# Moving eight of twelve attention chunks in between the matmul groups of the first expert layer

## The chip, the cores and the metric

The kernel runs on one core of one Trainium2 chip. The metric is the device time of one execution in microseconds (us); lower is better. All engines of the core run side by side, each through its own list of instructions: TensorE (PE, its weight loads are PEld), VectorE (DVE), ScalarE (ACT), GpSimd (POOL) and SyncE (SP), which here only issues DMAs. They are tied together by semaphores that the kernel sets and waits on by hand.

## What is computed

Three stages in a row, all in 32-bit floats. A gated recurrent attention (2 sequences, 8 heads, 768 steps, head size 40) gives rows `x` (1536 x 320), and two expert layers follow it, each a pair of 320 x 1536 projections multiplied with each other and a 1536 x 320 projection back:

```python
for t in range(S):
    m_new = np.maximum(f_gate[:, :, t] + m, i_gate[:, :, t])
    f_stab, i_stab = np.exp(f_gate[:, :, t] + m - m_new), np.exp(i_gate[:, :, t] - m_new)
    C = f_stab * C + i_stab * outer(vt, kt)        # one 40 x 40 state for each head
    n = f_stab * n + i_stab * kt
    y[:, :, t] = sigmoid(o_gate[:, :, t]) * (C @ qt) / max(|n . qt|, 1)
x = y as rows (1536 x 320)
x = (sigmoid(x @ w_gate) * (x @ w_val)) @ w_out    # first expert layer
x = ((x @ w_a) * (x @ w_b)) @ w_out2               # second expert layer
```

## The kernel before

**Attention.** The sequences are cut into chunks of 128 steps, 12 in all (`NCH`), numbered n = 2i + p with p the sequence. The gate sums and running maxima of all chunks are made at the start by DVE, on rows of 16 partitions (`gate_sums`, `gate_max`). For each chunk PE then makes these pieces:

- `spread` (L328): the weights' exponents of 8 heads, as 3 + 3 matmuls into a PSUM bank, one of each pair for the triangular mask (L340) and one that copies two rows of `arow` to all partitions (L350). The first chunk takes the rows from SBUF instead, with 8 small matmuls (L346).
- `scores` (L360): 3 matmuls, 1024 columns of f32.
- `from_state` (L370) and `values` (L381): the part out of the carried state `cst` and the part of the chunk itself, 8 small matmuls. They go into two banks, and DVE joins them.
- `to_state` (L393): what the chunk adds to the state.
- `turn` (L403): 3 transposes of the finished rows.

ACT makes `exp` of what `spread` wrote (`weigh`, L566), DVE multiplies with the scores (`product`, L768), joins the parts and divides (`combine`, L785 to L800), and updates the state (`state`, L775 and L778). POOL scales `v` (`weigh_v`, L894), decays the state (`decay`, L913) and multiplies with the opened output gate (`open_x`, L902 and L904). ACT and DVE then split the turned rows into a high and a low part in `xt` (`x_high` L189, `x_low` L194 and L196). The order on each engine is written out: in `step(i, p)` PE runs the first pieces of the next chunk around the last pieces of this one.

**Expert layers.** Each layer has 3 groups of 512 rows (`NG`) and 12 slices of the hidden size (`NF`): 72 units in both layers. In a unit, `up` makes two sums of 8 matmuls of 512 columns (L465), into `GB` and `VB`, which have two banks each; ACT (`gate`, L638 and L641) and DVE (`hidden`, L839 and L841) make of them `h_hi` and `h_lo`; `down` makes 12 matmuls of 320 columns (L482) into four banks `OB`. PE runs `up` of the next unit ahead of `down`. Between the layers the rows are copied to `x_next` and turned with 12 transposes a group (L513). The weights come as 24 tiles of 544 KB by DMA and are split into `w_hi` by ACT (L579, L586) and `w_lo` by POOL (L919). All tiles of the first layer are split in a fixed order from chunk 0 on; the first layer starts when the rows of the first four chunks are in `xt` (L531) and all but the end of the last chunk is done (L530 to L545).

Of the kernel before, what the change touches and what calls it, by code (L numbers as in the profile page):

```python
# [33 lines left out]
TRI = 3 * HD  # L34
KREM = DM - 2 * P
# [7 lines left out]
RING = 4  # L43
LATE = 5
EARLY = 6
THIRDS = ((0, 3), (3, 3), (6, 2))
LOW = -1.0e30
BIG = 2.0 ** 100


def wait(eng, sem, value):

    if not (isinstance(value, int) and value <= 0):
        eng.wait_ge(sem, value)


def build(nc, f_in, i_in, q_in, kq3_in, vk_in, o_in, w1_in, w2_in, consts_in, bm_in, out):
    ctx = ExitStack()
    with ctx:
# [5 lines left out]


# [8 lines left out]
        w_hi_late = sb("w_hi_late", [P, LATE * WC], F32R)  # L75
        w_hi = sb("w_hi", [P, (NF - LATE) * WC], F32R)
        w_lo = sb("w_lo", [P, EARLY * WC], F32R)
        opened = ExitStack()
        osig = opened.enter_context(nc.sbuf_tensor("osig", [P, NCH * DM], F32))
        opened.close()  # L80
        w_lo_late = sb("w_lo_late", [P, (NF - EARLY) * WC], F32R)
        xt = sb("xt", [P, 5 * TOK], F32R)
        w_raw0 = sb("w_raw0", [P, WC])
        consts = sb("consts", [P, 2 * P])
        ident = consts[:, 0:P]


        att = ExitStack()

        def ab(name, shape, dt=F32):  # L90
            return att.enter_context(nc.sbuf_tensor(name, shape, dt))

        q_blk = [ab(f"q_blk{i}", [TRI, HEADS * P]) for i in range(2)]
        k3 = [ab(f"k3_{i}", [TRI, 3 * P]) for i in range(2)]
        q3 = [ab(f"q3_{i}", [TRI, 3 * P]) for i in range(2)]
        arow = [ab(f"arow{i}", [P, HEADS * P], F32R) for i in range(2)]
        vk = [ab(f"vk_{i}", [P, VALL + 3 * TRI]) for i in range(2)]
        d_row = ab("d_row", [ROWS, CHUNKS])
        m_prev = ab("m_prev", [ROWS, CHUNKS])
        wt = ab("wt", [P, HEADS * P])  # L100
        pt = [ab(f"pt{i}", [P, HEADS * P]) for i in range(2)]
        u_num = ab("u_num", [P, VALL])
        x_raw = [ab(f"x_raw{i}", [P, DM]) for i in range(2)]
        x_n = [ab(f"x_n{i}", [P, 3 * P]) for i in range(2)]
        v_w = ab("v_w", [P, VALL])
        cst = [ab(f"cst{i}", [TRI, VALL]) for i in range(2)]
        t_st = ab("t_st", [TRI, VALL])
        bmask = ab("bmask", [TRI, VALL])
        g_col = ab("g_col", [P, NCH * HEADS])
        i_col = ab("i_col", [P, NCH * HEADS])  # L110
        w_col = ab("w_col", [P, NCH * HEADS])
        dec = ab("dec", [TRI, NCH * HEADS])
        den = [ab(f"den{i}", [P, HEADS]) for i in range(2)]
        rec = [ab(f"rec{i}", [P, HEADS]) for i in range(2)]
        ones = ab("ones", [P, P], F32R)
        consts_r = ab("consts_r", [P, 2 * P], F32R)
        ident_r, ahead = consts_r[:, 0:P], consts_r[:, P:2 * P]
        att.close()


        w_raw = [w_raw0, sb("w_raw1", [P, WC])]
        h_hi = [sb(f"h_hi{i}", [P, TG], F32R) for i in range(RING)]
        h_lo = [sb(f"h_lo{i}", [P, TG], F32R) for i in range(RING)]
        s_ff = [sb(f"s_ff{i}", [P, TG]) for i in range(2)]
        h_ff = [sb(f"h_ff{i}", [P, TG]) for i in range(2)]
        x_next = [sb(f"x_next{i}", [P, 3 * P]) for i in range(BLK)]
        y_out = [sb(f"y_out{i}", [P, DM]) for i in range(BLK)]

        bank = [ctx.enter_context(nc.psum_tensor(f"bank{i}", [P, 512], F32)) for i in range(8)]
        AB, OA, OI, SC, TP, ST = bank[0], bank[1], bank[4], bank[5], bank[6], (bank[2], bank[3], bank[7])  # L130
        GB, VB, OB = [bank[0], bank[2]], [bank[1], bank[3]], bank[4:8]

        a_dram = nc.dram_tensor("a_scratch", [2, CHUNKS * ROWS * P], F32, kind="Internal").ap()
        d_dram = nc.dram_tensor("d_scratch", [ROWS, CHUNKS], F32, kind="Internal").ap()

        (ld_gate, ld_ident, ld_bmask, st_rows, st_dec, ld_dec) = (
            sem(n) for n in ("ld_gate", "ld_ident", "ld_bmask", "st_rows", "st_dec", "ld_dec"))
        ld_o = [sem(f"ld_o{i}") for i in range(4)]
        ld_q, ld_a, ld_v = ([sem(f"ld_{x}{i}") for i in range(2)] for x in "qav")
        ld_w = [sem(f"ld_w{i}") for i in range(2)]  # L140
        (dve_gate, dve_split, dve_rows, dve_const, pe_cols, act_cols, act_osig, act_dec) = (
            sem(n) for n in ("dve_gate", "dve_split", "dve_rows", "dve_const", "pe_cols", "act_cols",
                             "act_osig", "act_dec"))
        (ab_ready, st_ready, act_exp, dve_p, pool_v, pe_av, pe_inter, pe_state) = (
            sem(n) for n in ("ab_ready", "st_ready", "act_exp", "dve_p", "pool_v", "pe_av",
                             "pe_inter", "pe_state"))
        (dve_t, pool_cd, dve_c, dve_u, dve_num, dve_den, dve_rec, dve_y, pool_x, pe_turn, act_xhi,
         dve_xlo) = (sem(n) for n in (
             "dve_t", "pool_cd", "dve_c", "dve_u", "dve_num", "dve_den", "dve_rec", "dve_y", "pool_x",
             "pe_turn", "act_xhi", "dve_xlo"))  # L150
        act_whi, pool_wlo, pool_zero, pool_lo = (
            sem(n) for n in ("act_whi", "pool_wlo", "pool_zero", "pool_lo"))
        (pe_g, pe_v, act_s, dve_h, act_hhi, dve_hlo, pe_mm2, pe_ob, act_next, dve_next, pe_tr, act_tr, dve_tr,
         act_y, dve_yo, st_out) = (sem(n) for n in (
             "pe_g", "pe_v", "act_s", "dve_h", "act_hhi", "dve_hlo", "pe_mm2", "pe_ob", "act_next", "dve_next",
             "pe_tr", "act_tr", "dve_tr", "act_y", "dve_yo", "st_out"))
# [11 lines left out]
        def w_part(low, f, at=0, k=WC):  # L168

            if low:  # L170
                tile, f = (w_lo, f) if f < EARLY else (w_lo_late, f - EARLY)
            else:
                tile, f = (w_hi, f) if f < NF - LATE else (w_hi_late, f - (NF - LATE))
            return tile[:, bass.ds(f * WC + at, k)]

        def w_buf(m, f):

            return 0 if m == 0 and f < EARLY else f % 2

        def w_landed(m, f):  # L180

            before = (EARLY if f % 2 == 0 else 0) + (NF - EARLY) // 2 * m
            return ld_w[f % 2], 16 * (before + (f - (EARLY if m == 0 else 0)) // 2 + 1)

        xt3 = xt[:, :].rearrange("p (j t) -> p j t", t=TOK)

        def split_high(act, bank_, at):

            return act.copy(xt3[:, 0::2, bass.ds(at, P)], bank_[:, 0:3 * P].rearrange("p (j t) -> p j t", t=P))  # L189
# [820 lines left out]
```

## Time and profile before

| | |
|---|---|
| median of 3 runs | 488.54 us (488.37 to 488.55) |
| the profiled execution | 488.71 us |
| its span, first to last instruction | 486.6 us |
| PE busy | 475.3 us (98%) |
| DVE, ACT, POOL busy | 190.9, 162.9, 95.6 us |
| moved by DMA | 28.90 MB, 59 GB/s over the span |

The page gives busy time as a share of the span. A PE that is busy all the time is not yet a PE at its peak, since matmuls are pipelined and their ends are modelled; so what a matmul costs is read from one start to the next. The profile's clock row (PEclk) is the share of the 2.4 GHz that was granted.

### The profile page before, as it was taken

The numbers are of one execution on the slowest core, as the hardware profiler recorded it, in microseconds if no ns is written. First come the engines' busy times: TensorE is split into PE (matmuls) and PEld (weight loads), VectorE is DVE, ScalarE is ACT, GpSimd is POOL, SyncE is SP. The second block draws the span as 40 slices with busy tenths as digits, with TensorE's granted clock in tenths as the row PEclk, the third lists the DMA queues.
The fourth block names the chain that finished last, engine by engine and source line by source line (L and its number), as shares of the span: only waits on it lengthen the run. The fifth ranks groups of instructions, "written<-read, shape, count | busy, mean of one in ns | idle before, by whom it ended". The sixth has DMA issues, their size and how long they took to land.

```text
span 486.6 us, 7131 instructions
## 1 busy us (share of the span) xinstructions
PE 475.3 (98%) x2587; PEld 417.3 (86%) x2587; DVE 190.9 (39%) x369; ACT 162.9 (33%) x320; POOL 95.6 (20%) x77
## 2 busy tenths in 40 slices
PE   4999999999999999999999999999999999999997
PEld 3788888888888888888988888888888888888886
DVE  8479999732222622224422235222232222222223
ACT  4555555434422422223333445222232222222222
POOL 1356666424500000000055443200000000000000
PEclk9999999999999999999999999999999999999999
DMA  7656655142310000000022331000010000100001
GB/s 253 173 167 180 191 189 165 46 139 90 95 47 0 2 0 1 0 1 0 1 92 93 100 129 49 1 0 1 0 55 0 1 0 1 54 1 1 1 0 54
DMA packets 15729, 28.90 MB, mean 59 GB/s; under 512 B 1850, under 2 KB 10530, under 8 KB 15702
## 3 DMA queue, kind: packets, MB, share of 16 engines
q1 hardware_dynamic: 15702, 28.53, 19.0%
q8 instruction: 18, 0.29, 0.3%
q14 instruction: 9, 0.07, 0.1%
HBM read 26.47 MB, written 2.05 MB: 59 GB/s over the span
## 4 chain that ended last, share of the span: by engine, by line
PE 93%; DVE 2%; DMA 1%; POOL 1%; issue 1%; SPq 1%; POOLq 0%; DVEq 0%
PE bank L465 54%; PE bank L482 26%; PE bank L381 3%; PE bank L360 3%; PE bank L370 1%; PE bank L393 1%; PE bank L340 1%; PE bank L403 1%; DMA q_blk<-q_in 1%; PE bank L350 1%; PE bank L513 1%; DVE m_row L722 1%; POOL w_lo L919 1%; POOL a_lo L926 0%; DMA d_scratch<-d_row 0%
## 5 line engine op out<-in xcount | busy, mean ns | idle before, releaser
L465 PE MATMUL bank<-xt,w_hi 128*128 128x512 f32 x420 | 137.5, 392 | 0.0
L839 DVE TENSOR_TENSOR h_ff<-bank,s_ff 128x512 f32<-128x512 f32 x72 | 49.8, 692 | 223.4 <-PE bank L465 211.3
L465 PE MATMUL bank<-xt,w_hi_late 128*128 128x512 f32 x300 | 97.9, 391 | 0.0
L641 ACT CAST h_hi<-h_ff 128x512 fp32r<-128x512 f32 x72 | 44.6, 620 | 143.6 <-DVE h_ff L839 143.6
L465 PEld LDWEIGHTS bank<-xt,w_hi 128*128 128x128 f32 x420 | 77.0, 188 | 13.9
L638 ACT ACTIVATE s_ff<-bank 128x512 f32<-128x512 f32 x72 | 43.1, 598 | 128.1 <-PE bank L465 128.0
L465 PE MATMUL bank<-xt,w_lo 128*128 128x512 f32 x216 | 84.1, 389 | 0.0
L465 PE MATMUL bank<-xt,w_lo_late 128*128 128x512 f32 x216 | 84.0, 389 | 0.0
L841 DVE TENSOR_TENSOR h_lo<-h_ff,h_hi 128x512 fp32r<-128x512 f32 x72 | 49.8, 692 | 49.3 <-ACT h_hi L641 49.3
L465 PEld LDWEIGHTS bank<-xt,w_hi_late 128*128 128x128 f32 x300 | 55.1, 188 | 9.9
L919 POOL TENSOR_TENSOR w_lo<-w_raw,w_hi 128x1088 fp32r<-128x1088 f32 (+1 forms) x12 | 31.5, 2622 | 122.7 <-ACT w_hi L586 122.7
L482 PE MATMUL bank<-w_hi,h_lo 128*128 128x320 f32 x168 | 51.9, 309 | 0.0
L482 PE MATMUL bank<-w_hi,h_hi 128*128 128x320 f32 x168 | 51.7, 308 | 0.0
L465 PEld LDWEIGHTS bank<-xt,w_lo 128*128 128x128 f32 x216 | 40.6, 188 | 8.8
L465 PEld LDWEIGHTS bank<-xt,w_lo_late 128*128 128x128 f32 x216 | 40.6, 188 | 8.7
L482 PE MATMUL bank<-w_lo,h_hi 128*128 128x320 f32 x144 | 44.4, 309 | 0.0
L482 PE MATMUL bank<-w_lo_late,h_hi 128*128 128x320 f32 x144 | 44.4, 309 | 0.0
L566 ACT ACTIVATE wt<-bank,g_col 128x128 f32<-128x128 f32 x96 | 28.6, 367 | 33.7 <-PE bank L350 32.5
L482 PE MATMUL bank<-w_hi_late,h_lo 128*128 128x320 f32 x120 | 37.1, 309 | 0.0
L482 PE MATMUL bank<-w_hi_late,h_hi 128*128 128x320 f32 x120 | 36.9, 308 | 0.0
L482 PEld LDWEIGHTS bank<-w_hi,h_hi 128*128 128x128 f32 x168 | 31.5, 188 | 1.4
L919 POOL TENSOR_TENSOR w_lo_late<-w_raw,w_hi_late 128x1088 fp32r<-128x1088 f32 x10 | 25.3, 2532 | 32.7 <-ACT w_hi_late L586 32.7
(88 smaller groups left out, 513.2 us busy)
## 6 DMA issues: line engine op xcount, KB each, us to landing
w_raw<-w_in SPq DMA_DIRECT2D x24, 544.0 KB, 3.6
vk<-vk_in SPq DMA_DIRECT2D x12, 344.0 KB, 3.4
k<-kq_in SPq DMA_DIRECT2D x12, 180.0 KB
q<-kq_in SPq DMA_DIRECT2D x12, 180.0 KB, 2.8
osig<-o_in SPq DMA_DIRECT2D x4, 480.0 KB, 5.4
y<-y_out SPq DMA_DIRECT2D x12, 160.0 KB, 1.8
q_blk<-q_in SPq DMA_DIRECT2D x24, 60.0 KB
q_blk<-q_in SPq DMA_DIRECT2D x12, 40.0 KB
```

Source lines behind the costliest of these rows:

```text
L340: pe.matmul(ab[:, 0:k * P], ident_r, ahead.unsqueeze(1).to_broadcast([P, k, P]), start=True, stop=False)
L350: pe.matmul(ab[:, 0:k * P], ones[:, :], arow[p][:, h * P:(h + k) * P], start=False, stop=True).then_inc(ab_ready, 1)
L360: pe.matmul(ST[x][:, 0:k * P], k3[p][:, x * P:(x + 1) * P], q_blk[p][:, h * P:(h + k) * P], start=True, stop=True).then_inc(st_ready, 1)
L381: mm = pe.matmul(OA[:, h * VW:(h + 1) * VW], pt[p][:, h * P:(h + 1) * P], vk[p][:, h * VW:(h + 1) * VW], start=True, stop=True)
L465: mm = pe.matmul(banks[f % 2][:, :], w_part(low, f, (gv * 3 + kt) * P, P), xt[:, bass.ds(xb * TOK + g * TG, TG)], start=(j == 0), stop=(j ...
L482: mm = pe.matmul(OB[tb][:, 0:DM], h[r][:, tb * P:(tb + 1) * P], w_part(low, f, W1C, DM), start=(f == 0 and j == 0), stop=(f == NF - 1 and ...
L566: a = act.activation(wt[:, h * P:(h + 1) * P], ab[:, j * P:(j + 1) * P], ACT.Exp, scale=-1.0, bias=g_col[:, bass.ds(n * HEADS + h, 1)])
L638: act.activation(s_ff[f % 2][:, :], GB[f % 2][:, :], fn).then_inc(act_s, 1)
L641: act.copy(h_hi[f % RING][:, :], h_ff[f % 2][:, :]).then_inc(act_hhi, 1)
L839: dve.tensor_tensor(h_ff[f % 2][:, :], VB[f % 2][:, :], s_ff[f % 2][:, :], ALU.mult).then_inc(dve_h, 1)
L841: dve.tensor_tensor(h_lo[f % RING][:, :], h_ff[f % 2][:, :], h_hi[f % RING][:, :].bitcast(F32), ALU.subtract).then_inc(dve_hlo, 1)
L919: pool.tensor_tensor(w_part(1, f), w_raw[0 if early else w_buf(m, f)][:, :], w_part(0, f).bitcast(F32), ALU.subtract).then_inc(pool_wlo, 1)
```

## The change

Four chunks (`ALONE`) run before the first expert layer starts, and the other eight are cut into three pieces each, which PE issues between the two halves of `up` and behind `down` in units 0 to 22 of the first layer's 36. One chunk takes three units. What else is different:

- `spread` is 2 matmuls of 512 columns: the mask stands in the rows of `arow` itself (filled once from `consts`), and a matrix `sel` picks them. The first chunk goes the same way, with its rows fetched by DMA.
- `q` is multiplied on POOL with a row of gate factors (`scale_q`, rows made by ACT in `i_rows`, stored to DRAM and fetched back three times over), so `from_state` and `values` add up in one bank, and `combine` on DVE has one product less and no sum.
- The gate factors' columns (`i_col`, one `columns` set of three) are gone.
- PSUM: `GB` and `VB` have one bank each, `OB` four, and two banks `XY` serve the pieces of attention. The SBUF tiles of one chunk exist once for the eight interleaved chunks and twice for the four alone.
- The output gate is opened for 4 chunks at once at the start, and for the others one by one.
- Every loop is unrolled; `w_raw` has three buffers; the weights are split at units given by `W_AT`.
- The next group's rows for the second layer are turned piecewise (`turn_rows`, at the units of `next_turns` and behind chunks 8 to 11), and `h_hi`, `h_lo` have two buffers in place of four.

The core of the diff: PE's pieces and order, then the order of ACT, of DVE and of POOL.

```diff
+UNITS = 2 * NG * NF
+ALONE = 4
+RING = 3
...
+def set_of(n):
+    return n % 2 if n < ALONE else 0
...
+def piece(u):
+    n, k = divmod(u + 1, 3)
+    n += ALONE
+    return (n, k) if n < NCH else (None, None)
...
+        GB, VB, OB, XY = bank[0], bank[1], bank[2:6], bank[6:8]
...
+            def spread(n):
+                s = set_of(n)
+                pe.wait_ge(ld_a[s], 32 + 16 * use_of(n))
+                for half in range(2):
+                    if n <= ALONE:
+                        wait(pe, act_e, 2 * n - 1 + half)
+                    elif half == 0:
+                        pe.wait_ge(dve_xlo, n)
+                    else:
+                        wait(pe, dve_c, n if last_with_state(n - 1) else 0)
+                        wait(pe, dve_tr, n - 8)
+                    pe.matmul(XY[half][:, :], sel[:, :], arow[s][:, half * HALF:(half + 1) * HALF],
+                              start=True, stop=True).then_inc(pe_ab, 1)
...
+            def values(n):
+                s, p = set_of(n), n % 2
+                acc = value_bank(n)
+                if n >= BATCH:
+                    pe.wait_ge(dve_y, n - 1)
+                    pe.wait_ge(dve_c, n - 1)
+                    pe.wait_ge(pool_q, n - 1)
+                    if n >= ALONE:
+                        pe.wait_ge(dve_p, 2 * n + 1)
+                    for x, (h, k) in enumerate(((0, 3), (3, 3), (6, 2))):
+                        mm = pe.matmul(acc[:, h * VW:(h + k) * VW], q3[s][:, x * P:(x + 1) * P],
+                                       cst[p][:, h * VW:(h + k) * VW], start=(x == 0), stop=False)
+                    mm.then_inc(pe_f, 1)
...
+            spread(1)
+            scores(1, 0)
+            scores(1, 1)
+            values(0)
+            columns(range(1, CHUNKS), 0, dve_gate, 9)
+            columns(range(1, CHUNKS), 1, dve_rows, 3)
+            to_state(0)
+            spread(2)
+            scores(2, 0)
+            scores(2, 1)
+            pe.wait_ge(act_cols, 4)
+            turn(0)
+            values(1)
+            to_state(1)
+            spread(3)
+            scores(3, 0)
+            scores(3, 1)
+            turn(1)
+            values(2)
+            spread(4)
+            values(3)
+            to_state(2)
+            to_state(3)
+            scores(4, 0)
+            turn(2)
+            scores(4, 1)
+            turn(3)
...
+            for u in range(UNITS - 1):
+                n, k = piece(u)
+                up(u, 0)
+                if k == 0:
+                    spread(n)
+                if k == 1 and n > ALONE:
+                    scores(n, 0)
+                    scores(n, 1)
+                if k == 2 and last_with_state(n):
+                    to_state(n)
+                up(u, 1)
+                if k == 2:
+                    turn(n)
+                    if n >= NCH - BLK:
+                        turn_rows(0, n - (NCH - BLK))
+                for g, tb in next_turns(u):
+                    turn_rows(g, tb)
+                if u == UNITS - 2:
+                    up(u + 1, 0)
+                    up(u + 1, 1)
+                if u:
+                    down(u - 1)
+                if k == 1:
+                    values(n)
...
+            weigh(0, 0)
+            weigh(0, 1)
+            i_rows()
+            weigh(1, 0)
+            weigh(1, 1)
+            w_high(0)
+            gate_cols(1)
+            act.wait_ge(ld_dec, 16)
+            act.activation(dec[:, :], dec[:, :], ACT.Exp).then_inc(act_dec, 1)
+            act.wait_ge(act_cols, 3)
+            weigh(2, 0)
+            weigh(2, 1)
+            x_high(0)
+            w_high(1)
+            weigh(3, 0)
+            weigh(3, 1)
+            x_high(1)
+            w_high(2)
+            weigh(4, 0)
+            weigh(4, 1)
+            x_high(2)
+            x_high(3)
+            w_high(3)
...
+            W_AT = {0: (4,), 1: (5, 6), 3: (7,), 4: (8, 9), 6: (10,), 7: (11,)}
+            for u in range(UNITS):
+                n, k = piece(u)
+                gate(u)
+                if k == 0:
+                    weigh(n, 0)
+                if k == 1:
+                    open_gate(n)
+                h_high(u)
+                if k == 0:
+                    weigh(n, 1)
...
+            state(0)
+            product(2, 0)
+            product(2, 1)
+            x_low(0)
+            combine(1)
+            state(1)
+            product(3, 0)
+            product(3, 1)
+            x_low(1)
+            combine(2)
+            combine(3)
+            state(2)
+            state(3)
+            product(4, 0)
+            x_low(2)
+            x_low(3)
+            product(4, 1)
...
+            for u in range(UNITS):
+                n, k = piece(u)
+                if k == 1 and n > ALONE:
+                    product(n, 0)
+                    product(n, 1)
+                if k == 2:
+                    combine(n)
+                    if last_with_state(n):
+                        state(n)
+                hidden(u)
+                h_low(u)
...
+            pool.wait_ge(act_cols, 2)
+            weigh_v(0)
+            weigh_v(1)
+            w_low(0)
+            open_x(0)
+            pool.wait_ge(act_cols, 4)
+            scale_q(2)
+            weigh_v(2)
+            w_low(1)
+            open_x(1)
+            decay(2)
+            scale_q(3)
+            weigh_v(3)
+            open_x(2)
+            decay(3)
+            open_x(3)
+            w_low(2)
+            scale_q(4)
+            weigh_v(4)
+            w_low(3)
```

SP issues its DMAs one after the other too. Ahead of the interleaved part its order is: gate rows, constants, output gate, `q`, `v` of chunk 0, `q` of chunk 1, the four `arow` rows of chunks 0 and 1 (which wait for the masks and for DVE), `v` of chunk 1, the mask, weight tile 0; then the stores of the exponent rows (after POOL's `a_lo`), the store of the gate factors (after ACT's `i_rows`), `q` and the rows of chunk 2, the store and the fetch of the decays (`dec`) with the scaled `q` of chunk 2 between them, and `v` 2, rows and `q` 3, tile 1, and so on.

## Rows read from the trace of the kernel before

**Rows 1.** The page's first part: busy us, share of the span and instructions.
```profile
PE 475.3 (98%) x2587; PEld 417.3 (86%) x2587; DVE 190.9 (39%) x369; ACT 162.9 (33%) x320; POOL 95.6 (20%) x77
```

**Rows 2.** Timeline of PE in the attention stage: start us, us, what.
```profile
31.62 1.89 PE L360 MATMUL bank<-q_blk,k 120*128 120x384 f32 x6
33.16 0.53 PE L340 MATMUL bank<-consts_r 128*128 128x384 f32 x1
```

**Rows 3.** Timeline of PE at the start of the first expert layer.
```profile
86.79 0.70 PE L465 MATMUL bank<-xt,w_hi 128*128 128x512 f32 x2
...
87.56 0.62 PE L465 MATMUL bank<-xt,w_hi 128*128 128x512 f32 x2
...
88.71 0.79 PE L370 MATMUL bank<-cst,q 120*128 120x123 f32 x6
89.34 1.92 PE L381 MATMUL bank<-vk,pt 128*128 128x41 f32 x16
91.08 0.53 PE L403 MATMUL bank<-consts,x_n 128*128 128x128 f32 x3
```

**Rows 4.** Chain of work that ended last: start us, us, what; attention, then expert units.
```profile
31.78 1.72 PE bank L360 x6
...
104.59 3.65 PE bank L465 x16
108.24 1.75 PE bank L482 x12
...
162.31 1.31 PE bank L513 x12
```

**Rows 5.** Timelines of DVE and of POOL at the start.
```profile
4.83 0.41 DVE L713 TENSOR_TENSOR_SCAN s_row<-rst,f_row 16x128 f32<-16x128 f32 x1
...
12.95 0.48 DVE L753 CAST a_hi<-m_row 16x640 fp32r<-16x640 f32 x1
...
13.51 2.12 POOL L926 TENSOR_TENSOR a_lo<-m_row,a_hi 16x640 fp32r<-16x640 f32 x1 [10.93 <-DVE a_hi L753]
```

**Rows 6.** DMA from 15 to 40 us: what, size, median us to landing.
```profile
w_raw<-w_in SPq DMA_DIRECT2D x2, 544.0 KB, 4.3
...
dec<-d_scratch SPq DMA_DIRECT2D x1, 45.0 KB, 3.8
```

**Rows 7.** Timeline of ACT.
```profile
13.05 2.17 ACT L566 ACTIVATE wt<-bank,g_col 128x128 f32<-128x128 f32 x8
...
30.17 1.10 ACT L579 CAST w_hi<-w_raw 128x1088 fp32r<-128x1088 f32 x1
...
92.20 1.28 ACT L638 ACT_TABLE_LOAD   x1
```

**Rows 8.** Timelines of DVE and of POOL in one chunk.
```profile
64.64 0.17 DVE L792 SCALAR_TENSOR_TENSOR den<-u_num 128x8 f32<-128x8 f32 x1
...
65.79 0.55 DVE L768 TENSOR_TENSOR pt<-bank,wt 128x384 f32<-128x384 f32 x1
66.26 0.41 DVE L194 TENSOR_TENSOR xt<-bank,xt 128x256 f32 x1
...
67.01 0.92 DVE L768 TENSOR_TENSOR pt<-bank,wt 128x384 f32<-128x384 f32 x2
...
66.06 0.32 POOL L902 TENSOR_TENSOR x_n<-x_raw,osig 128x64 f32<-128x64 f32 x1 [2.85 <-DVE x_raw L800]
66.35 0.87 POOL L904 TENSOR_TENSOR x_n<-x_raw,osig 128x320 f32<-128x320 f32 x1
```

**Rows 9.** Timelines of POOL and of DVE at 70 us.
```profile
69.08 2.75 POOL L919 TENSOR_TENSOR w_lo<-w_raw,w_hi 128x1088 f32 x1
...
70.46 1.41 DVE L792 SCALAR_TENSOR_TENSOR den<-u_num 128x8 f32<-128x8 f32 x1
```

**Rows 10.** Timeline of PE at 13 us, and busy time by stretch at the end.
```profile
13.27 3.78 PE L360 MATMUL bank<-q_blk,k 120*128 120x384 f32 x6
...
484.50:486.60 2.10, 0.00 (x0) 0.00 (x0) 0.00 (x0) 0.00 (x0) 0.00 (x0) 0.71 0.50 173
```

More of the change, by code:

```diff
@@ L294, in _ @@
[L294 to L307 removed]
+            sp.dma_start(dec[:, :], d_dram.rearrange("r c -> (r c)").partition_broadcast(TRI)).then_inc(ld_dec, 16)
@@ new lines, in scores @@
+            def scores(n, half):
+                s = set_of(n)
+                pe.wait_ge(ld_q[s], 64 * (use_of(n) + 1))
+                if n < ALONE:
+                    wait(pe, dve_p, 2 * n - 1 + half)
+                elif n == ALONE:
+                    pe.wait_ge(dve_y, n - 1 + half)
+                else:
+                    pe.wait_ge(act_e, 2 * n + half + 1)
+                st = score_bank(n, half)
+                for h, k in (((0, 3), (3, 1)), ((4, 2), (6, 2)))[half]:
+                    at = (h - half * HEADS // 2) * P
+                    x = h // 3
+                    mm = pe.matmul(st[:, at:at + k * P], k3[s][:, x * P:(x + 1) * P],
+                                   q_blk[s][:, h * P:(h + k) * P], start=True, stop=True)
+                mm.then_inc(pe_s, 1)
@@ L548, in _ @@
-            run(0, NG - 1, after_turn(NG - 1), 0, "next")
-            run(1, 0, after_turn(NG), 1, True)
-            with pe.Fori(1, NG - 1) as g:
-                run(1, g, after_rows(g), g + 1, False)
-            run(1, NG - 1, after_rows(NG - 1), None, False)
+                mm.then_inc(pe_d, 1)
+            pe.wait_ge(ld_ident, 16)
+            columns(range(1), 0, dve_gate, 5)
+            columns(range(1), 1, dve_rows, 1)
+            scores(0, 0)
+            scores(0, 1)
+            pe.wait_ge(pool_sel, 4)
@@ L872, in _ @@
[L872 to L884 removed]
+            product(1, 0)
+            product(1, 1)
+            combine(0)
+            dve.wait_ge(ld_bmask, 16)
@@ new lines, in _ @@
+            for u in range(3 * (NCH - ALONE) - 1):
+                n, k = piece(u)
+                if k == 0 and n > ALONE:
+                    scale_q(n)
+                    if last_with_state(n):
+                        weigh_v(n)
+                if k == 2:
+                    if last_with_state(n):
+                        decay(n)
+                    open_x(n)
+                for f in W_AT.get(u, ()):
+                    w_low(f)
+            for f in range(NF):
+                w_low(NF + f)
```

1065 lines of the change are left out of this document (443 added, 622 removed).

## The prediction, made before the changed kernel was run

> **What bounds the kernel now.** I read the page's first part first. PE is busy 475.3 of 486.6 us, the other engines at most 191 [rows 1]. So only what PE executes, or a wait of PE, can move the end. The timeline of PE then shows two regimes. Up to 86.8 us it runs the twelve chunks, each piece starting where the one before ends [rows 2]; from there on it runs expert units with no gap [rows 3], and in the chain that ended last each unit takes 3.65 + 1.75 = 5.40 us [rows 4]. Seventy-two of them are 389 us, which the change does not touch: same matmuls, same columns. What is open is the attention, and what the reader has to ask is two things: how much PE time eight chunks cost inside the units, and when the first unit can start if only four chunks, with nothing beside them, stand ahead of it.
>
> **What stays.** From 86.79 to the end of the span are 399.8 us. In it stand one `from_state` (88.71 to 89.34, 0.63), one chunk of `values` (89.34 to 91.08, 1.74) and two turns (91.08 is followed by the next unit 0.3 later, so 0.27 each) [rows 3]. Without them 396.9 us remain: the units, three times 1.31 for the turned rows between the layers [rows 4], and the stores at the end.
>
> **What the eight chunks add inside the units (on the path).** A `spread` is now two matmuls of 512 columns. Sixteen such matmuls take 3.65 [rows 4], so 0.23 each, 0.46. `scores` keep 1024 columns of f32: 1.72 [rows 4], against 1.54 from start to start [rows 2]; I take 1.75, since there are four pairs of instructions in place of three. `from_state` and `values` are 0.63 + 1.70, `to_state` has the six instructions of `from_state` and I take 0.67, a turn 0.27. Seven chunks (5 to 11) cost 4.81 each, 33.7; five of them also a `to_state`, 3.3; chunk 4, whose `spread` and `scores` run ahead, 3.3. Sum 40.3. A unit that starts behind f32 work has its first two matmuls 0.08 us longer (0.70 against 0.62 [rows 3]); with four such seams a chunk that is 0 to 2.9 us, and I take 2.6.
>
> Waits inside the units: with one bank each, `up` of unit u into `GB` must wait for ACT's sigmoid of unit u-1, but between them PE has the second half of `up` (1.83) and a `down` (1.75), 3.6 us for an ACT instruction of 0.6. `VB` is the same with `hidden`. The turn at the end of a chunk needs `combine` (1.15, 64.64 to 65.79) and `open_x` (0.32 + 0.87) [rows 8]: 2.4 us behind the end of `values`, while PE has 4.3 us of work. Only in the first of these units is POOL late, behind `w_low` of tile 4, which itself waits for ACT: 0.5 us. The two banks `XY` are free by the same margins. ACT has to change between the tables of exp and sigmoid about fifteen times, 1.28 us each [rows 7]; it has 21 us for a chunk's three units and uses half, and the `h_hi` that follows an exp is needed 5 us later. I cost that at nothing; if the cover were gone it would be 15 times 1.28, 19 us.
> The Trainium skill ("ScalarE: Activation LUTs", section "What ACT_TABLE_LOAD costs") puts a switch at 2.66 us, with a drain behind the load. By that price the `h_hi` is still 4 us early, and the sum stays. The row shows the load alone.
>
> **When the first unit starts.** This decides. I lay the orders of the four engines and of SP side by side with the lengths of the rows.
> DVE no longer fills `arow` and `cst` before the gate rows; those land 1.9 us after their issue, near 3.2, so the scan that started at 4.83 [rows 5] starts at 3.2. The chain behind it is 0.4 shorter too: `a_hi` at 11.0 to 11.5 in place of 12.95, and POOL's `a_lo` (2.12) ends at 13.6 [rows 5]. That gain of 2 us is then spent by SP. The fetch of `dec` stands behind the stores, `q` 2, the rows and the four DMAs of `scale_q`: about 19.2 against 18.7 before, and with 3.8 to land [rows 6] it is there at 23.0. ACT waits for it in front of the exps of chunk 2, and POOL in front of `scale_q` 2. Before 23.3 everything else has room: `scores` 0 from 7.4 to 10.7, the first exps at 11.3 (13.05 before), chunk 1 complete but for its state.
> From 23.3: exps of chunk 2, 2.2 [rows 7], and `x_high` 0, 26.0; `w_high` 1, 1.1 [rows 7], 27.2; POOL's `w_low` 1, 2.7 [rows 9], 29.8; `open_x` 1, 1.2 [rows 8], 31.0. PE has been idle since 27.5, because turn 1 stands ahead of `values` 2 in its list: 3.6 us. Then turn 1, `values` 2 (2.33), `spread` 4 and `values` 3 end at 36.5, `combine` 3 at 37.6, `state` 2 needs 1.0 plus 0.6 (below) to 39.2, `to_state` 3 to 39.9, the product of `state` 3 to 40.4, its sum to 42.1 (below), product 4, `x_low` 2 (0.7, from 66.26 [rows 8]), turn 3, `x_high` 3, `x_low` 3: 45.1.
> What is "below": a short DVE instruction with both inputs in SBUF took 1.41 us and ended when POOL's `w_low` ended (70.46 + 1.41 against 69.08 + 2.75) [rows 9]. So DVE's sum of two SBUF tiles in `state` 2 meets `open_x` 3, and that of `state` 3 meets `w_low` 2: 0.6 and 1.2 us, and they stand in the chain.
> The Trainium skill has this as a rule ("SBUF — State Buffer", section "Who interferes with whom": two SBUF inputs on VectorE against a GpSimd instruction that reads SBUF exclude each other for the whole instruction). It adds that `combine`, which now reads PSUM and one SBUF tile, is not held; by the row alone one could fear 1.2 us there too, which would give 46.3 in place of 45.1.
>
> **The clock.** At 13.27 six instructions of `scores` took 3.78 us, at 31.62 the same six 1.89 [rows 2, 10]: PE began at half its clock and got the full one only behind dense score matmuls, near 17 us, though it had been executing small matmuls since 7 us. At the other end the granted clock is 0.71 on average from 484.50 to 486.60, so it fell about 2 us after the last matmul [rows 10]. The kernel before never idles in between. The changed one idles 3.6 us before turn 1 and is then less than half busy from 36.5 to 45.1. I expect a fall to 1.2 GHz there. Bounds: nothing, if it holds; if it falls at 31 and comes back only in the expert units, `values` 2 and 3 double (+4.7), the rest of the chain gets 1.3 longer, and the first units lose 2: 8.0. I take 4.0, the middle, since dense `values` stand right behind the gap and no row tells whether they bring the clock back.
>
> **Sum.** 396.9 + 40.3 + 2.6 + 0.5 + 45.1 + 4.0 = 489.4 us of span. The profiled execution took 488.71 for 486.6, 2.1 more, and the median is 0.2 below it: 489.4 + 2.1 - 0.2 = 491.3. The gain on PE is real (about 0.9 us less `spread` for each chunk, 6 at the first), but the four chunks alone leave PE idle for 12 to 13 us, and before they left none.
>
> **Rivals.**
> - The clock holds. All else the same, 485.4 of span, 487.3. For it: the four chunks have matmuls in every few us up to 27.5. Against: the row of the end, 2 us without work. It is near no change, and with an error of 2.5 us in the hand schedule it falls on both sides.
> - The handovers overlap better than I laid them out, and the change is faster. Its place is the stage of four chunks: `dec` lands by 20.3 (3.0 earlier), `w_low` 1 is not in the way of `open_x` 1 (1.8), and the two holds by POOL don't meet (1.2). Then the first unit starts at 39.1: 485.4 - 6.0 = 479.4 of span, 481.3. For it: each is a matter of order and of a landing time that the trace shows for another load. Against: the order is written out in the diff, and SP, ACT and POOL keep it. It decides from about 3 us of the 6 on.
> - The pieces hold up the units: a piece waits on DVE or POOL behind PE's own order, and `up` behind it. With 0.4 us in each of 23 units, 9 us come on top: 500. For it: single banks. Against: the margins of 1.5 to 3 us above.
> - It does what it says but gains nothing, since PE was full already: this is in the first rival.
>
> **How the numbers follow.** Forecast 0.46, clock holds 0.28, better overlap 0.18, held units 0.08. About 0.2% (1 us) is what a measurement of this kernel can tell from no change: faster is below 487.5, slower above 489.5. The forecast's own range is 487.3 to 495.3: 0.06 of it is same, 0.40 slower. Clock holds: 0.17 faster, 0.08 same, 0.03 slower. Better overlap: faster. Held units: slower. That gives 0.35, 0.14, 0.51. The range goes from just below the better overlap, 480.0, to the forecast's upper bound with 1 us for the seams and the schedule, 496.5; outside are the held units and the ends of the others.
>
> **What would show it.** The first matmul of the expert layer starts near 45 to 50 us (86.79 before). PE has an idle stretch of 3 to 4 us that ends with POOL's `x_n` of chunk 1, and ACT's exps of chunk 2 start right behind `dec`. The granted clock is below 1 somewhere from 27 to 50 us. From there to the end are some 438 to 442 us without PE waits over 0.5 us. `h_lo` stays at 0.69 us except where POOL splits weights. The sum is wrong in its first term if the units take other than 5.40 us; the forecast is wrong if the first unit starts before 43 us, or if the clock stays at 1 throughout.

## The result and the profile after

The changed kernel takes 497.22 us (median of 4, 496.81 to 497.53) beside 488.55 us of the kernel before (488.37 to 488.58): 1.0178 times as long, with an interval of 1.016 to 1.0195. It is slower by 8.7 us. 491.3 was predicted with a range up to 496.5, so the direction was right and the time lies 0.7 us outside the range.

The first parts of the page of the changed kernel, where the lines of PE and PEclk answer to [rows 1]:

```profile
span 495.7 us, 6537 instructions
PE 474.7 (96%) x2532; PEld 415.7 (84%) x2532; DVE 172.5 (35%) x338; ACT 182.6 (37%) x344; POOL 103.9 (21%) x88
PE   3858899999999999999999999999999999999997
...
PEclk9985899999999999999999999999999999999999
```

PE's busy time is what it was (474.7 against 475.3), though each chunk's `spread` has less to do. Part of it is the same work done at half the clock: the one digit of PEclk under 8 is the fourth slice, 37 to 50 us. The timeline of PE in that stretch (start, duration, in brackets the idle time before and what ended it; [rows 2, 3] are the same view of before):

```profile
27.80 2.00 PE L398 MATMUL bank<-q_blk,k 120*128 120x384 f32 x8 [0.26 <-DMA q_blk<-q_in]
34.19 0.90 PE L443 MATMUL bank<-consts,x_n 128*128 128x128 f32 x3 [4.40 <-POOL x_n L927]
...
36.09 3.55 PE L419 MATMUL bank<-vk,pt 128*128 128x41 f32 x16
...
48.13 1.49 PE L432 MATMUL bank<-v_w,vk 128*120 128x123 f32 x6 [1.65 <-DVE cst L790]
...
55.71 0.70 PE L484 MATMUL bank<-xt,w_hi 128*128 128x512 f32 x2 [1.38 <-issue]
...
59.45 0.79 PE L413 MATMUL bank<-cst,q 120*128 120x123 f32 x6
60.08 1.92 PE L419 MATMUL bank<-vk,pt 128*128 128x41 f32 x16
```

PE idles 4.40 us before turn 1 (L443). `values` (L419) take 3.55 at 36.09 and 1.92 at 60.08, for the same 16 matmuls. The first expert unit (L484) starts at 55.71. The granted clock says why the lengths differ (stretch, its length, PE busy and instructions, PEclk, DMA share, GB/s):

```profile
31.00:33.00 2.00, 0.00 (x0) 1.00 1.03 347
33.00:34.00 1.00, 0.00 (x0) 0.83 1.00 261
...
36.00:45.00 9.00, 9.00 (x43) 0.50 0.15 43
45.00:53.00 8.00, 6.35 (x23) 0.50 0.49 156
...
54.00:55.00 1.00, 0.32 (x2) 0.93 0.35 48
```

The clock falls to its lower level, 1.2 GHz, during the idle stretch, and stays there for 20 us, through 9 us in which PE is busy all the time. Behind 60 us the clock holds and PE hardly waits:

```profile
60.00:495.70 435.70, 432.51 (x2339) 1.00 0.15 47
```

The clock is 1.00, and the waits of PE from there to the end hold one entry, 0.3 us (`x_n` of chunk 4). So the loss lies wholly ahead of the first unit.

One caution on the clock row. It reads 1.00 from the start of the trace, also for 7.00 to 14.00, though PE runs at half its speed for most of that: the same eight `scores` instructions take 3.78 us in chunk 0 and 1.90 in chunk 1 (timeline of PE). What the row and the mean clocks below show is the time behind the first rise only.

```profile
8.55 3.78 PE L398 MATMUL bank<-q_blk,k 120*128 120x384 f32 x8 [2.06 <-DMA q_blk<-q_in]
...
15.42 1.90 PE L398 MATMUL bank<-q_blk,k 120*128 120x384 f32 x8
```

What made PE wait for turn 1 is seen on ACT (same columns as PE's timeline) ...

```profile
24.64 0.28 ACT L676 ACTIVATE dec<-dec 120x96 f32<-120x96 f32 x1 [4.48 <-DMA dec<-d_scratch]
24.83 2.15 ACT L585 ACTIVATE wt<-bank,g_col 128x128 f32<-128x128 f32 x8
26.83 0.53 ACT L200 CAST xt<-bank 128x384 fp32r<-128x384 f32 x1
29.39 1.10 ACT L613 CAST w_hi<-w_raw 128x1088 fp32r<-128x1088 f32 x1 [2.03 <-DMA w_raw<-w_in]
```

... on POOL ...

```profile
30.56 2.48 POOL L948 TENSOR_TENSOR w_lo<-w_raw,w_hi 128x1088 fp32r<-128x1088 f32 x1 [3.82 <-ACT w_hi L613]
33.00 0.32 POOL L926 TENSOR_TENSOR x_n<-x_raw,osig_a 128x64 f32<-128x64 f32 x1
33.28 0.86 POOL L927 TENSOR_TENSOR x_n<-x_raw,osig_a 128x320 f32<-128x320 f32 x1
```

... and on SP's queue, where tile 1 stands behind the fetches of chunks 2 and 3:

```profile
23.05 1.15 SPq L257 DMA_DIRECT2D q_blk<-q_in  x3
24.24 0.35 SPq L287 DMA_DIRECT2D w_raw<-w_in  x1
```

DVE had `x_raw` of chunk 1 ready at 29.8; POOL took it up at 33.00, straight behind `w_lo`. The chain is: tile 1 issued at 24.24, landed about 29.3, split by ACT to 30.49, by POOL to 33.04, then `open_x`, then turn 1.

### The profile page after: what moved, and what is told of

Same layout as the page of the kernel before. It is cut to its first block, busy times and chain, and to the rows that moved or that the text cites. A ratio compares the mean times of both kernels' runs of the same rounds, so it can differ in the third digit from the quotient of the medians.

```text
span 495.7 us, 6537 instructions
## 1 busy us (share of the span) xinstructions
PE 474.7 (96%) x2532; PEld 415.7 (84%) x2532; DVE 172.5 (35%) x338; ACT 182.6 (37%) x344; POOL 103.9 (21%) x88
## 4 chain that ended last, share of the span: by engine, by line
PE 91%; issue 3%; POOL 2%; DMA 2%; SPq 1%; ACT 1%; DVE 0%; POOLq 0%; DVEq 0%; ACTq 0%
PE bank L484 52%; PE bank L501 26%; PE bank L398 4%; PE bank L419 4%; PE bank L413 1%; PE bank L432 1%; PE bank L443 1%; PE bank L381 1%; DMA q_blk<-q_in 1%; PE bank L466 1%; POOL w_lo L948 1%; DMA dec<-d_scratch 1%; POOL x_n L927 0%; POOL q_blk L952 0%; ACT wt L585 0%
## 5 line engine op out<-in xcount | busy, mean ns | idle before, releaser
L484 PE MATMUL bank<-xt,w_hi 128*128 128x512 f32 x360 | 118.6, 394 | 1.4 <-issue 1.4
L635 ACT ACTIVATE s_ff<-bank 128x512 f32<-128x512 f32 x72 | 43.1, 599 | 136.4 <-PE bank L484 136.4
L484 PE MATMUL bank<-xt,w_lo 128*128 128x512 f32 x216 | 84.7, 392 | 0.0
L484 PEld LDWEIGHTS bank<-xt,w_hi 128*128 128x128 f32 x360 | 65.6, 188 | 13.4 <-issue 1.7
L484 PE MATMUL bank<-xt,w_hi_mid 128*128 128x512 f32 x180 | 59.3, 394 | 0.0
L484 PE MATMUL bank<-xt,w_hi_end 128*128 128x512 f32 x180 | 59.3, 394 | 0.0
L484 PEld LDWEIGHTS bank<-xt,w_lo 128*128 128x128 f32 x216 | 40.5, 188 | 8.8
L948 POOL TENSOR_TENSOR w_lo<-w_raw,w_hi 128x1088 fp32r<-128x1088 f32 x12 | 30.5, 2545 | 59.6 <-ACT w_hi L613 59.6
L484 PE MATMUL bank<-xt,w_lo_mid 128*128 128x512 f32 x108 | 42.4, 393 | 0.0
L484 PE MATMUL bank<-xt,w_lo_end 128*128 128x512 f32 x108 | 42.3, 392 | 0.0
L484 PEld LDWEIGHTS bank<-xt,w_hi_end 128*128 128x128 f32 x180 | 33.0, 188 | 6.0
L484 PEld LDWEIGHTS bank<-xt,w_hi_mid 128*128 128x128 f32 x180 | 32.9, 188 | 5.9
L585 ACT ACTIVATE wt<-bank,g_col 128x128 f32<-128x128 f32 x96 | 26.8, 369 | 7.2 <-PE bank L381 7.1
L398 PE MATMUL bank<-q_blk,k 120*128 120x256 f32 (+2 forms) x96 | 26.7, 425 | 2.3 <-DMA q_blk<-q_in 2.3
L501 PEld LDWEIGHTS bank<-w_lo,h_hi 128*128 128x128 f32 x144 | 27.1, 189 | 1.2
```

Of the source, the lines that this page charges most:

```text
L398: mm = pe.matmul(st[:, at:at + k * P], k3[s][:, x * P:(x + 1) * P], q_blk[s][:, h * P:(h + k) * P], start=True, stop=True)
L484: mm = pe.matmul(up_bank(u, gv)[:, :], w_part(low, f, (gv * 3 + kt) * P, P), xt[:, xb * TOK + g * TG:xb * TOK + (g + 1) * TG], start=(j == ...
L501: mm = pe.matmul(OB[tb][:, 0:DM], h[r][:, tb * P:(tb + 1) * P], w_part(low, f, W1C, DM), start=(f == 0 and j == 0), stop=(f == NF - 1 and ...
L585: a = act.activation(wt[:, at:at + P], XY[half][:, h * P:(h + 1) * P], ACT.Exp, scale=-1.0, bias=g_col[:, col:col + 1])
L635: act.activation(s_ff[u % 2][:, :], up_bank(u, 0)[:, :], ACT.Sigmoid if u < UNITS // 2 else ACT.Copy).then_inc(act_s, 1)
L948: pool.tensor_tensor(w_part(1, j % NF), w_raw[j % RING][:, :], w_part(0, j % NF).bitcast(F32), ALU.subtract).then_inc(pool_wlo, 1)
```

## The experiments

All times below are medians beside the kernel before on the same chip. In the summary, "behind" is the span less the start of the first unit; each row is the profiled execution.

| kernel | turn 1 | first unit | behind | span | mean clock |
|---|---|---|---|---|---|
| predicted | 31.1 | 45.1, with the clock 49.1 | 440.3 | 489.4 | |
| the change | 34.19 | 55.71 | 440.0 | 495.7 | 0.979 |
| gaps filled, 128 rows | 34.98 | 49.63 | 440.0 | 489.6 | 0.997 |
| gaps filled, 16 rows | 35.34 | 61.13 | 441.4 | 502.5 | 0.969 |
| `open_x` 1 ahead of `w_low` 1 | 31.36 | 50.64 | 441.6 | 492.2 | 0.985 |
| `dec` early | 34.14 | 55.31 | 440.0 | 495.3 | 0.976 |
| tiles 1 and 2 behind attention | 30.91 | 47.36 | 440.0 | 487.4 | 0.986 |
| tiles late, `dec` early, gaps and start filled | 34.04 | 48.61 | 440.0 | 488.6 | 0.986 |
| the same, nine more fills at the start | 32.11 | 46.05 | 440.1 | 486.1 | 0.996 |
| one table load in the units | 34.07 | 55.24 | 441.6 | 496.8 | 0.975 |

**Is it the clock, and what holds it?** Two kernels put unused matmuls of 512 columns into the gaps, alike but for the number of rows that they read (the second passes `ROWS`, 16, in place of `P`, 128).

```diff
+            def fill(bank_, k, rows=P):
+                for _ in range(k):
+                    pe.matmul(bank_[:, :], w_part(0, 0, 0, P)[0:rows, :], w_part(0, 0, 0, 512)[0:rows, :],
+                              start=True, stop=True)
...
             scores(3, 1)
+            pe.wait_ge(act_whi, 1)
+            pe.wait_ge(dve_xlo, 1)
+            fill(bank[5], 18, P)
             turn(1)
...
+            pe.wait_ge(dve_xlo, 2)
+            fill(bank[5], 7, P)
             to_state(3)
...
+            pe.wait_ge(dve_c, 4)
+            fill(bank[4], 5, P)
             turn(3)
```

> The changed kernel with idle PE time filled: 18 matmuls of 128 rows x 512 columns ahead of turn 1, 7 ahead of to_state 3, 5 ahead of turn 3, all into free banks and used by nobody. Theory (the fallen clock costs the time): the granted clock stays at 1 from 15 us on, values 2 and 3 take 2.3 us each in place of 4.5, the first expert unit starts near 48 us in place of 55.7, and the time is about 489.5 us. Rival (the handovers between POOL, DVE and ACT set the start, and a slow PE only uses idle time): the first unit starts within 1 us of 55.7, time 496 to 498. If the extra matmuls themselves push PE back, up to 500.

> As the dense fill, but each of the 30 matmuls reads 16 rows in place of 128, with the same columns, so PE is just as busy. If being busy keeps the clock, this is as fast as the dense fill (about 489.5). If the clock goes by how much of the array works, as the slow start of the kernel before suggests (PE busy with 16-row matmuls from 7 us, full clock only near 17 us), the clock falls at 33 to 34 us as in the changed kernel and the time stays near 497.

With 128 rows the median is 494.8 us (491.38 to 498.69, ratio 1.0144, 1.0076 to 1.0213). The single executions fall into two pairs: spans of 489.6 and 490.0 with mean clocks of 0.997 and 1.0, and 496.0 and 496.9 with 0.979 and 0.99. So the filling holds the clock in some executions only, and the mean clock does not order them all: the longest span goes with 0.99, not with 0.979, so something else varies too, which one trace a kernel does not show. The profiled one is of the first pair (timeline of PE):

```profile
30.03 4.46 PE L511 MATMUL bank<-w_hi 128*128 128x512 f32 x18
34.98 0.55 PE L443 MATMUL bank<-consts,x_n 128*128 128x128 f32 x3 [0.49 <-POOL x_n L941]
...
35.99 1.92 PE L419 MATMUL bank<-vk,pt 128*128 128x41 f32 x16
...
49.63 0.70 PE L484 MATMUL bank<-xt,w_hi 128*128 128x512 f32 x2 [1.38 <-issue]
```

The order of the work is that of the change; `values` take 1.92 and the first unit starts 6.1 us earlier. With 16 rows, in the same place and as long:

```profile
30.10 5.31 PE L511 MATMUL bank<-w_hi 16*128 16x512 f32 x18
35.34 0.90 PE L443 MATMUL bank<-consts,x_n 128*128 128x128 f32 x3
...
37.24 3.55 PE L419 MATMUL bank<-vk,pt 128*128 128x41 f32 x16
```

and its clock by stretches:

```profile
31.00:32.00 1.00, 1.00 (x6) 1.00 0.97 334
32.00:34.00 2.00, 2.00 (x9) 0.82 1.09 301
34.00:45.00 11.00, 11.00 (x48) 0.50 0.30 82
```

PE has no gap here, and the clock falls nearly where it fell in the idle stretch of the change. The kernel is the slowest of all, 503.06 us (1.0286, 1.0256 to 1.0317), since the filling itself runs at half the clock in the chain. A PE that the page calls busy can still be granted 1.2 GHz. That the number of rows is what separates the two kernels is borne out by the profiles, but since two of the dense one's four executions are as long as the change, and the thin one was timed twice, it is not proved.

**What makes turn 1 late?** One kernel opens chunk 1 before it splits tile 1; another fetches `dec` ahead of the factors' rows and lets DVE run the products of chunk 0 behind the rows that `dec` needs.

```diff
+            open_x(1)
             w_low(1)
-            open_x(1)
```

> The changed kernel with one swap on POOL: open_x of chunk 1 ahead of w_low of tile 1, which waits for the tile's DMA (landed at 29.3). Theory: turn 1 runs near 31.1 in place of 34.2, PE's gap is 1.3 us in place of 4.4. If a shorter gap keeps the clock up to 37 us, values 2 and 3 are at full speed and the first unit starts at 46 to 49: 488 to 490.5. If the clock falls anyway, only the 3.1 us of the wait come back: 494. Rival (POOL's order is hidden): 497.

```diff
+            sp.wait_ge(dve_rows, 2)
+            sp.dma_start(d_dram, d_row[:, :]).then_inc(st_dec, 16)
...
+            sp.wait_ge(st_dec, 16)
+            sp.dma_start(dec[:, :], d_dram.rearrange("r c -> (r c)").partition_broadcast(TRI)).then_inc(ld_dec, 16)
...
-            sp.wait_ge(dve_rows, 2)
-            sp.dma_start(d_dram, d_row[:, :]).then_inc(st_dec, 16)
...
-            sp.wait_ge(st_dec, 16)
-            sp.dma_start(dec[:, :], d_dram.rearrange("r c -> (r c)").partition_broadcast(TRI)).then_inc(ld_dec, 16)
...
+            dve.tensor_tensor(d_row[:, :], m_prev[:, :], by3(m_row, 0, CHUNKS)[:, :, P - 1],
+                              ALU.subtract).then_inc(dve_rows, 1)
             product(0, 0)
             product(0, 1)
-            dve.tensor_tensor(d_row[:, :], m_prev[:, :], by3(m_row, 0, CHUNKS)[:, :, P - 1],
-                              ALU.subtract).then_inc(dve_rows, 1)
```

> The changed kernel with the decays' store and fetch issued ahead of the gate factors' store, q 2 and the scaled q 2 (dec landed at 24.6; here about 19 to 20). Theory (tile 1, landing at 29.3, and the clock decide): the exps of chunk 2 start 3 to 4 us earlier, but w_high 1 still waits for its tile, so 0 to 1 us gained, 496 to 497. Rival (dec is the head of the chain, as the prediction had it): 3 us gained, 494.

The early `dec` does what it should on ACT, where the exps of chunk 2 start at 22.45 in place of 24.83. Then ACT waits longer for the tile:

```profile
22.45 2.17 ACT L585 ACTIVATE wt<-bank,g_col 128x128 f32<-128x128 f32 x8 [0.61 <-PE bank L381]
...
29.34 1.10 ACT L613 CAST w_hi<-w_raw 128x1088 fp32r<-128x1088 f32 x1 [4.19 <-DMA w_raw<-w_in]
```

Turn 1 stays at 34.14 and the time at 497.88 us (1.0197, 1.017 to 1.0223). So `dec` does not set turn 1. With `open_x` 1 first, turn 1 comes at 31.36 and the gap is 0.76 us; the clock is kept through `values` 2 and falls later (timeline of PE):

```profile
32.37 1.92 PE L419 MATMUL bank<-vk,pt 128*128 128x41 f32 x16
...
36.40 0.87 PE L413 MATMUL bank<-cst,q 120*128 120x123 f32 x6 [1.27 <-POOL q L934]
37.10 3.36 PE L419 MATMUL bank<-vk,pt 128*128 128x41 f32 x16
```

The kernel takes 494.69 us (1.0113, 1.0066 to 1.016), 3.2 less than the one with the early `dec` on the same chip; 494 was expected for a clock that falls all the same. It falls once more in the first unit, where it reads 0.50 from 51 to 54 us, and that is why 441.6 us lie behind the start of that unit here. In the next kernel tiles 1 and 2 stand further back on both engines:

```diff
-            w_high(1)
             weigh(3, 0)
             weigh(3, 1)
             x_high(1)
-            w_high(2)
+            w_high(1)
             weigh(4, 0)
             weigh(4, 1)
+            w_high(2)
...
-            w_low(1)
             open_x(1)
-            decay(2)
             scale_q(3)
             weigh_v(3)
+            decay(2)
+            w_low(1)
             open_x(2)
             decay(3)
             open_x(3)
-            w_low(2)
             scale_q(4)
             weigh_v(4)
+            w_low(2)
```

> The changed kernel with the weight tiles 1 and 2 moved behind the attention on ACT (w_high 1 behind x_high 1, w_high 2 behind the exps of chunk 4) and on POOL (open_x 1, scale_q 3, v 3 and the decay 2 ahead of w_low 1; w_low 2 behind v 4). Theory (the wait for tile 1 opens the gap in which the clock falls): turn 1 near 31, no gap over 1.5 us up to 37, values 2 and 3 at full speed in most executions, first unit at 46 to 48 us: 488 to 490. If the clock still falls from 37 us on, where PE is less than half busy, the first unit starts at 49 to 51: 491 to 493. Rival (the tile's place does not matter): 497.

It takes 489.82 us (1.0034, 1.0004 to 1.0065): turn 1 at 30.91 behind a gap of 0.20, `values` 2 and 3 at 1.92 and 1.95, the first unit at 47.36. The clock still falls, at 15, at 22 and at the end of the stage, there behind the gap of 1.70 before `to_state` 3. At 22 PE had been busy without a gap since 15.06 (stretches, columns as above):

```profile
20.00:23.00 3.00, 3.00 (x23) 0.83 0.65 128
23.00:25.00 2.00, 2.00 (x7) 0.50 0.79 251
...
38.00:39.00 1.00, 0.03 (x1) 1.00 0.32 76
39.00:44.00 5.00, 4.28 (x15) 0.51 0.77 247
```

**Do the pieces in the units cost more than their matmuls?** In the changed kernel 15 table loads stand in the units (L585 and L635, lines and counts of ACT):

```profile
L635 ACT ACT_TABLE_LOAD x8 | 10.3, 1283 | 0.1
L585 ACT ACT_TABLE_LOAD x7 | 9.0, 1283 | 0.1
```

The next kernel uses the sigmoid in place of the exponential for chunks 5 to 11, so their weights are left out of the computation and ACT changes its table only once, for the first unit.

```diff
-                    a = act.activation(wt[:, at:at + P], XY[half][:, h * P:(h + 1) * P], ACT.Exp, scale=-1.0,
+                    a = act.activation(wt[:, at:at + P], XY[half][:, h * P:(h + 1) * P], ACT.Exp if n <= ALONE else ACT.Sigmoid, scale=-1.0,
```

> The changed kernel with the exponentials of chunks 5 to 11 replaced by sigmoid, so that their result is left out and ACT never changes its table in the units. Theory (the fourteen table loads are hidden behind PE): from the first unit to the end 440.0 us as in the changed kernel, time within 1 us of 497.2. Rival (they hold gate and h_hi, and PE behind them): up to 18 us less, 479.

One load of the 15 is left, and the time is 498.53 us (1.0199, 1.0182 to 1.0216), no shorter. Its 441.6 us behind the first unit's start against 440.0 are one piece at the start: the clock there was 0.63 and 0.50 up to 59 us. From chunk 4's product with the state, behind that piece, both kernels take 436.2 us to the end (59.45 to 495.7 in the change, 60.58 to 496.8 here). The loads are hidden.

**Can the stage be mended?** This kernel joins the early `dec`, the late tiles and three fills (6, 7 and 5 matmuls), and adds 15 dense matmuls around the first small ones.

```diff
+            pe.wait_ge(dve_ones, 1)
+            warm(bank[2], 6)
             pe.wait_ge(ld_ident, 16)
             columns(range(1), 0, dve_gate, 5)
+            warm(bank[2], 4)
             columns(range(1), 1, dve_rows, 1)
+            warm(bank[2], 5)
             scores(0, 0)
```

> The order of e5_no_tile_wait, the decays early as in e4_dec_early, dense unused matmuls in the gaps as in e1_dense_fill (6, 7 and 5), and 15 unused matmuls at the start so that PE is at its full clock when the scores of chunk 0 come. Theory: granted clock 1 from about 8 us on, scores 0 in 1.7 us in place of 3.3, first unit near 43 to 45 us, time 484 to 487, faster than the kernel before. If only the clock counted in the changed kernel and the handovers stay, 489.

It is the first that beats the kernel before, by little: 487.22 us (484.91 to 493.6, 10 executions), 0.9962 (0.9943 to 0.9982). The profiled execution, one of the long ones, shows one reason: the clock fell at 13.3, where PE had been idle for 2.2 of 2.9 us, and `scores` 1 took 3.62 us (timeline of PE). It stayed at 0.50 to 26.9, through all of `scores` 1 and `values` 0, with PE busy.

```profile
13.36 0.77 PE L382 MATMUL bank<-arow,sel 128*128 128x512 f32 x1 [1.16 <-ACT wt L609]
...
14.90 3.62 PE L399 MATMUL bank<-q_blk,k 120*128 120x384 f32 x8
```

The last kernel fills that place too.

```diff
             scores(0, 1)
+            warm(bank[3], 3)
             pe.wait_ge(pool_sel, 4)
             spread(0)
+            warm(bank[3], 5)
             spread(1)
+            warm(bank[3], 1)
```

> Adds to the kernel with all gaps filled nine more unused matmuls of 512 columns by 128 rows: three behind the scores of chunk 0, five behind its spread, one behind the spread of chunk 1. There, from 10.5 to 13.4 us, PE idled for 2.2 us of 2.9 and the granted clock fell to 0.5 at 13.3 and stayed there until 26.9. If gaps between dense matmuls are what takes the clock, it now stays at 1 from 8 us on, the first unit starts near 45 (48.6 in the kernel with the same gaps filled from 27 us on), the span is 485 and the median some 2 to 3 us under 487.2, with less spread between executions. Rival: once the clock holds, what sets the start is only the chain of landings (dec, tile 1) and the end of the handovers of chunk 3; then the clock is 1 and the first unit still starts at 48 to 49, time unchanged. A third: the clock falls at another place in spite of the filling, near 38 to 45 us.

486.63 us (484.63 to 487.84), 0.9942 (0.9925 to 0.9959), the best of all. Its early stage:

```profile
14.64 1.90 PE L399 MATMUL bank<-q_blk,k 120*128 120x384 f32 x8
...
27.33 3.56 PE L399 MATMUL bank<-q_blk,k 120*128 120x384 f32 x8 [1.70 <-DMA q_blk<-q_in]
```

`scores` 1 are back at 1.90, the first unit starts at 46.05, and what is left is one loss behind a wait of 1.70 us for `q_blk` (27.33: 3.56 us). Of its executions, three with mean clocks of 0.999 to 1.0 have spans of 482.8 to 484.7, and three with 0.996 have 484.9 to 486.1. Its distance to the kernel before it in the table, 0.6 us of median where 2 to 3 were expected, is within what both scatter.

**Would the kernel before gain by the same means?** Twelve dense matmuls go ahead of its first small ones.

```diff
+            pe.wait_ge(dve_const, 1)
+            for _ in range(12):
+                pe.matmul(ST[0][:, :], ones[:, :], ones[:, :].unsqueeze(1).to_broadcast([P, 4, P]),
+                          start=True, stop=True)
```

> The kernel before with 12 unused dense matmuls on PE ahead of its first work, from 1 to 6 us. It started with PE at half its clock up to near 17 us. Theory (thin matmuls do not hold the clock): the masks and row copies of chunk 0 from 7.2 to 13.3 keep it up only in part, so between 0 and 3 us gained, 485.5 to 488.5. Rival (PE's early work is hidden behind other waits): no change, 488.5 to 489.

```profile
11.80 3.78 PE L360 MATMUL bank<-q_blk,k 120*128 120x384 f32 x6
...
25.77 3.50 PE L360 MATMUL bank<-q_blk,k 120*128 120x384 f32 x6 [1.00 <-DMA q_blk<-q_in]
```

No: 489.97 us (1.0023, 1.0004 to 1.0041), where 485.5 to 488.5 was expected. `scores` 0 start at 11.80 in place of 13.27 [rows 10] but at half the clock (0.80 on average from 6 to 11 us, 0.50 from 11 to 15), which had fallen again during the small matmuls, most of them of 16 rows, and the earlier start ran into the landing of `q_blk`, behind which the clock fell once more.

## Why the prediction was right or wrong

The predicted span was 489.4 and the measured one 495.7, 6.3 longer. The table of the experiments gives the parts: turn 1 late 3.1, the clock 2.9 more than taken, the rest of the chain 0.65, the part behind the first unit 0.3 less; together 6.35.

- **What stays, and the eight chunks in the units: right.** 440.3 was predicted and 440.0 came. The terms hold one by one: from a `spread` to the next (70.71, 92.70, 114.70) are 22.0 us; less three units of 5.40 that is 5.8 for a chunk, and 4.81 + 0.67 + four seams of 0.08 is 5.8. POOL was late once, 0.3 us where 0.5 was taken. So the rival of pieces that hold up the units fell, and so did the fear of the table loads. The price of a switch on the Trainium skill's page ("ScalarE: Activation LUTs", section "What ACT_TABLE_LOAD costs"), 2.66 us, could not be told from 1.28 here, since both are covered; the load alone is 1.283 in the trace, 15 times.
- **The schedule up to turn 1: wrong by 3.1 us.** The failed step is "Before 23.3 everything else has room". It had `scores` 0 end at 10.7, but they waited for `q_blk` and ran from 8.55 to 11.8; the exps of chunk 0 started at 12.86 in place of 11.3, and the orders of ACT and SP passed that on to `dec`, which landed near 24.6, not 23.0. And it gave tile 1 no time of landing. Tile 1 was issued at 24.24, and landed 5 us later under a DMA load of some 300 GB/s. ACT waited 2.03 us for it (the cast itself takes 1.10, as in [rows 7]), and the kernel with `dec` early shows that it is the tile, not `dec`, that sets turn 1; with the tile out of the way turn 1 came at 30.91. That turn 1 stands behind `w_low` 1 in POOL's order was seen; that this made PE wait for a weight tile was not. The idle time of PE ahead of the first unit, put at 12 to 13 us and none before, was 17.9 (55.71 less 37.85 busy) and 8.0 before (86.79 less 78.75); it is no term of the sum.
- **The chain from turn 1: right to 0.65 us.** 14.0 was predicted at full clock; the filled kernel took 14.65 (34.98 to 49.63). Its five fills ahead of turn 3 hardly lengthen that: turn 3, at 47.73, also waits for DVE's `x_low` 2, which ended at 47.58 (last line below). Port holds are in it as predicted in kind: DVE's sum of `state` took 1.13 and 1.08 us there against 0.50 where POOL was idle (at 87.68 and 109.69 in the change), 1.2 together where 1.8 was taken, as by the rule of the Trainium skill cited in the prediction ("SBUF — State Buffer", section "Who interferes with whom"); in the change it was 0.86 and 0.50, and at the 0.50 DVE was first and POOL's `scale_q` took 1.33 in place of 1.00. `combine`'s product was never held (0.490 to 0.492, 12 times, one of them beside `w_lo` 0), as that page of the Trainium skill says.

```profile
42.51 1.13 DVE L804 TENSOR_TENSOR cst<-cst,t_st 120x328 f32<-120x328 f32 x1
44.65 0.50 DVE L801 TENSOR_TENSOR t_st<-bank,bmask 120x328 f32<-120x328 f32 x1 [1.02 <-PE bank L432]
45.26 1.08 DVE L804 TENSOR_TENSOR cst<-cst,t_st 120x328 f32<-120x328 f32 x1
...
47.29 0.29 DVE L207 TENSOR_TENSOR xt<-bank,xt 64x128 fp32r<-64x128 f32 x1
```

(DVE in the kernel with the dense fills; L801 reads PSUM, L804 two tiles in SBUF, L207 ends `x_low`.)
- **The clock: the mechanism right, the size wrong.** It fell in the predicted gap, and 4.0 was taken, between 0 and 8.0. From turn 1 to the first unit the change needs 21.5 us and the filled kernel 14.65: 6.9. Up to the start of `to_state` 2 it is 5.1 (10.80 against 5.68; 4.7 in the upper bound), behind it 1.75 (1.3). The 2 us for the first units did not come in the change, since the clock was back before 55; in the three kernels with 441.4 to 441.6 behind the first unit's start they came, as 1.4 to 1.6. The failed clause is that "dense `values` stand right behind the gap" and might bring the clock back: PE ran from turn 1 through `values` 3 for 10.8 us without a gap, all of it at 1.2 GHz. The bound was built rightly; its middle had no row behind it. The range gave the schedule 1 us beside the clock's bound of 8.0, while the schedule was 3.75 us late; so it ended 0.7 us short (495.3 and 1 are 496.3, not the 496.5 that was written).
- **The rival of better overlap fell for the change, but its list was the way to mend it.** `open_x` ahead of `w_low` gave 2.8 us at turn 1 by itself. With the tiles out of the way the change comes to 1.0034, and with `dec` early and all fills as well to 0.9942, 2.5 us better than before. The rival in which the clock holds fell, since the clock fell in all four executions (0.976 to 0.979). Its 487.3 would not have come either: the filled kernel, at a mean clock of 0.997, takes 491.38, since turn 1 is late in it all the same.

## What to carry to other kernels

When work that kept the engine full is moved elsewhere, lay out the stage that remains with every transfer in it, also those that serve a later stage: here a weight tile for the experts held up a turn of attention, through POOL's order. Put such splitting behind the work that PE waits for, not ahead of it. Then price a gap on PE with its consequence. The trace of the kernel before already had the same `scores` at both clocks (3.78 and 1.89 us), and here the lower clock was paid on all the work of the stage from the gap on, 20 us, not on the piece behind the gap alone.

## What was not expected of the hardware

- The granted clock stayed at 0.50 through 9.00 us of 9.00 busy (36 to 45 us) with matmuls of 41 and 123 columns and two of 512, and came back just behind 54. In the kernel with 16-row fills, and at 22 us in the one with the tiles late, it fell with PE busy in every slice around it.
- Filling is not safe. The same kernel, with the same instructions, had spans of 489.6 and 496.9, with mean clocks of 0.997 and 0.99. The clock is part of that; the rest is open.
- Why the clock in the change returned when it did, during turn 3 and behind `scores` 4, no run here explains. It came back during or behind `scores` 4 in four other kernels too (at 47.5, 53.4, 45.9 and 52.4 us), but `scores` 1 in the kernel with all gaps filled did not bring it back. No run tests what does.
